# The up projection by seven block products instead of eight, in tiles of 1024 tokens

## The chip, the cores and the metric

The kernel runs on one core of a Trainium2 chip. The metric is the device time of one execution in microseconds (us). Engines are named as the profile names them: PE is TensorE (PEld its weight loads), DVE is VectorE, ACT is ScalarE, POOL is GpSimd, SP is SyncE, which issues the DMAs.

## What is computed

```python
def _attn_ref(x, f_logit, lower_bound):          # x: (2, 6080, 256)
    sig = 1.0 / (1.0 + np.exp(-f_logit))
    f = lower_bound + (1.0 - lower_bound) * sig
    i = 1.0 - f
    for t in range(S):
        h = f[:, t] * h + i[:, t] * x[:, t]
        y[:, t] = h

def _moe_ref(x, w_in, w_out):                    # 12160 tokens, 256 -> 2048 -> 256
    h = x @ w_in
    relu6 = np.clip(h + 3.0, 0.0, 6.0)
    return (h * relu6 / 6.0) @ w_out
```

A gated scan over the tokens of each of two sequences gives the states; they go through an up projection, a gate and a down projection. The inputs are float32.

## The kernel before

Channels lie on the partitions, tokens along the free dimension. The 256 channels are two groups of 128 (k = 0, 1), the 2048 hidden units sixteen blocks f of 128, the output channels two groups d. A tile is 512 tokens of one of the two sequences b (448 in each sequence's first tile), 24 tiles in all, the sequences taking turns.

To keep float32 accuracy with matmuls that round their operands, each operand is split in two: ACT casts it to the rounded type (`_hi`), and a subtraction gives the rest (`_lo`). A product is then three matmuls: hi x hi, hi x lo, lo x hi. So a tile has for each f 2 x 3 matmuls up (`up`, L436, matmuls on L449) and 2 x 3 down (`down`, L455, L469).

For each tile DVE and ACT make the states: sigmoid on ACT (L316), forget gate, drive and scan on DVE (L341, L346, L353), the cast on ACT (L321), the rest on POOL (L245, one pass over both groups). For each f, ACT clips h from below (L267, `clipped`, reads PSUM), DVE clips it from above and multiplies it with h (L363, `g`, one input in SBUF, one in PSUM), ACT casts g (L272), and DVE makes the rest (L368, both inputs in SBUF). At the tile's end ACT copies y out of PSUM (L328) and SP stores it.

PSUM holds four banks of h (`h_ps`, `SLOTS`) and four of y. The order of the work on each engine is written out by hand: TensorE does down(f) of a tile and then up(f + 4), so that four h banks lie between its two uses, and a result of `up` has about three f to pass through ACT and DVE. The work for the next tile's states is put at f = 0 to 5. Each engine takes its instructions strictly in this order; a wait on a semaphore holds everything behind it. SP loads tile t + 2 once tile t's x and z are read, from buffers for both sequences.

At the start the weights come in eight pieces of two f each and are split: casts on ACT (L258, L262), rests of w_in on DVE and POOL (L336, L235), of w_out on POOL (L229); 28 small matmuls on zeros run ahead of the first real one. The loop over the tiles is a hardware loop except for the first two and the last two tiles.

## Time and profile before

| | |
|---|---|
| median of 3 runs | 1053.38 us (1053.21 to 1053.45) |
| the profiled execution | 1055.17 us, span of its trace 1053.2 us |
| instructions | 12791, of them 4636 matmuls (28 on zeros) |
| granted TensorE clock | 0.998 of 2.4 GHz |
| DMA | 41.74 MB, 40 GB/s |
| ACT idle until a result of `up` | 504.1 us |
| DVE idle until ACT's clip | 418.2 us |

The page gives busy time and its share of the span for each engine, then the span in 40 equal slices, then a chain of waits followed back from the last instruction, then groups of instructions by line with the mean length of one in ns, the idle time of the engine just before them, and who ended it. The timeline lists instructions by start and length, with the idle time before them and its releaser in brackets.

### The profile page before, as it was taken

What the parts mean: (1) busy time and instruction counts of PE and PEld (TensorE: products, weight loads), DVE (VectorE), ACT (ScalarE), POOL (GpSimd) and SP (SyncE); (2) the same over time, 40 slices, a digit from 0 to 9 for tenths busy, and PEclk for the clock granted to TensorE, in tenths of its full rate; (3) what the DMA queues carried; (4) which work ended last, traced back from release to release, by engine and by line L of the source; (5) the groups of instructions that cost most, each with busy time, mean ns of one, the idle gap of its engine ahead of it and who ended that gap; (6) DMA issues with size and microseconds to landing.
All of it is one profiled execution on the core that took longest, in us unless ns stands there. A gap on an engine that the chain in (4) does not pass through costs nothing.

```text
span 1053.2 us, 12791 instructions
## 1 busy us (share of the span) xinstructions
PE 1044.3 (99%) x4636; PEld 870.5 (83%) x4636; DVE 623.8 (59%) x950; ACT 533.7 (51%) x859; POOL 70.7 (7%) x37
## 2 busy tenths in 40 slices
PE   7999999999999999999999999999999999999998
PEld 6998888888888888888888888888888888888887
DVE  7864665656646566465665656646556465564644
ACT  5655444544545545455454554544545544454443
POOL 3300000000000000000000000000000000000000
PEclk9999999999999999999999999999999999999999
DMA  7011010110101101011010110101101011010000
GB/s 270 1 58 44 15 61 0 60 59 1 60 0 60 60 0 60 0 60 60 0 60 0 60 60 0 60 0 60 60 0 60 17 43 60 0 60 21 1 21 20
DMA packets 22093, 41.74 MB, mean 40 GB/s; under 512 B 1600, under 2 KB 3136, under 8 KB 22080
## 3 DMA queue, kind: packets, MB, share of 16 engines
q1 hardware_dynamic: 22080, 41.56, 11.6%
q8 instruction: 9, 0.15, 0.1%
q14 instruction: 4, 0.03, 0.0%
HBM read 29.10 MB, written 12.45 MB: 39 GB/s over the span
## 4 chain that ended last, share of the span: by engine, by line
PE 98%; DVE 0%; ACT 0%; issue 0%; ACTq 0%
PE y_ps L469 49%; PE h_ps L449 49%; DVE state L353 0%; DVE state_lo L383 0%; ACT clipped L267 0%; DVE g_lo L368 0%; DVE g L363 0%; DVE drive L346 0%; ACT y_sb L328 0%; ACT g_hi L272 0%; ACT state_hi L281 0%; ACTq L266 0%
## 5 line engine op out<-in xcount | busy, mean ns | idle before, releaser
L267 ACT ACTIVATE clipped<-h_ps,half 128x512 f32<-128x512 f32 (+1 forms) x384 | 263.1, 685 | 504.1 <-PE h_ps L449 504.1
L363 DVE SCALAR_TENSOR_TENSOR g<-clipped,h_ps 128x512 f32<-128x512 f32 (+1 forms) x384 | 262.1, 683 | 418.5 <-ACT clipped L267 418.2
L449 PE MATMUL h_ps<-state_hi,w_in_hi 128*128 128x512 f32 (+1 forms) x768 | 298.3, 388 | 3.5 <-DVE state_lo L383 3.0
L469 PE MATMUL y_ps<-g_hi,w_out_hi 128*128 128x512 f32 (+1 forms) x768 | 297.4, 387 | 1.0 <-DVE g_lo L368 1.0
L449 PE MATMUL h_ps<-state_lo,w_in_hi 128*128 128x512 f32 (+1 forms) x768 | 298.1, 388 | 0.0
L449 PE MATMUL h_ps<-state_hi,w_in_lo 128*128 128x512 f32 (+1 forms) x768 | 298.0, 388 | 0.0
L469 PE MATMUL y_ps<-g_hi,w_out_lo 128*128 128x512 f32 (+1 forms) x768 | 297.4, 387 | 0.0
L469 PE MATMUL y_ps<-g_lo,w_out_hi 128*128 128x512 f32 (+1 forms) x768 | 297.4, 387 | 0.0
L368 DVE TENSOR_TENSOR g_lo<-g,g_hi 128x512 fp32r<-128x512 f32 (+1 forms) x384 | 273.4, 712 | 0.2
L272 ACT CAST g_hi<-g 128x512 fp32r<-128x512 f32 (+1 forms) x384 | 233.3, 608 | 1.2 <-DVE g L363 1.1
L449 PEld LDWEIGHTS h_ps<-state_hi,w_in_hi 128*128 128x128 f32 x768 | 144.5, 188 | 33.2 <-DVE state_lo L383 3.0
L469 PEld LDWEIGHTS y_ps<-g_hi,w_out_hi 128*128 128x128 f32 x768 | 144.1, 188 | 30.0 <-issue 1.3
L449 PEld LDWEIGHTS h_ps<-state_hi,w_in_lo 128*128 128x128 f32 x768 | 144.5, 188 | 28.8
L449 PEld LDWEIGHTS h_ps<-state_lo,w_in_hi 128*128 128x128 f32 x768 | 144.4, 188 | 28.6
L469 PEld LDWEIGHTS y_ps<-g_lo,w_out_hi 128*128 128x128 f32 x768 | 144.2, 188 | 28.9
L469 PEld LDWEIGHTS y_ps<-g_hi,w_out_lo 128*128 128x128 f32 x768 | 144.2, 188 | 28.5
L245 POOL TENSOR_TENSOR state_lo<-state,state_hi 128x1024 fp32r<-128x1024 f32 (+1 forms) x23 | 55.4, 2407 | 885.7 <-ACT state_hi L321 885.7
L353 DVE TENSOR_TENSOR_SCAN state<-gate,carry,drive 128x512 f32<-128x512 f32 (+1 forms) x48 | 61.7, 1286 | 0.2
L346 DVE SCALAR_TENSOR_TENSOR drive<-sig,one_minus_lb,x_sb 128x512 f32<-128x512 f32 (+1 forms) x48 | 35.6, 741 | 1.3 <-DMA x_sb<-in_x 1.3
L328 ACT COPY y_sb<-y_ps 128x1024 f32<-128x1024 f32 (+2 forms) x24 | 23.8, 993 | 3.4 <-PE y_ps L469 3.4
L321 ACT CAST state_hi<-state 128x1024 fp32r<-128x1024 f32 (+1 forms) x23 | 24.1, 1048 | 0.7 <-DVE state L353 0.7
L316 ACT ACTIVATE sig<-z_sb 128x1024 f32<-128x1024 f32 (+1 forms) x23 | 24.4, 1059 | 0.0
(23 smaller groups left out, 76.8 us busy)
## 6 DMA issues: line engine op xcount, KB each, us to landing
z_sb<-in_z SPq DMA_DIRECT2D x22, 512.0 KB, 4.6
x_sb<-in_x SPq DMA_DIRECT2D x22, 512.0 KB, 5.2
out_y<-y_sb SPq DMA_DIRECT2D x21, 512.0 KB, 3.2
w_in_raw<-in_w_in SPq DMA_DIRECT2D x8, 256.0 KB, 6.2
w_out_raw<-in_w_out SPq DMA_DIRECT2D x8, 256.0 KB, 7.4
out_y<-y_sb SPq DMA_DIRECT2D x2, 448.0 KB, 3.3
out_y<-y_sb SPq DMA_DIRECT2D x2, 256.0 KB, 2.1
z_sb<-in_z SPq DMA_DIRECT2D x2, 224.0 KB, 3.5
```

The lines of the kernel that those rows point to most:

```text
L245: nc.gpsimd.tensor_tensor(state_lo[:, nb, :, 0:n], state[:, :, 0:n], state_hi[:, nb, :, 0:n].bitcast(F32), ALU.subtract).then_inc(state_lo ...
L267: nc.scalar.activation(clipped[:, s, 0:n], h_ps[:, s, 0:n], ACT.Relu, bias=half[:], scale=1.0 / 6.0).then_inc(clipped_ready, 1)
L272: nc.scalar.copy(g_hi[:, s, 0:n], g[:, s, 0:n]).then_inc(g_hi_ready, 1)
L316: nc.scalar.activation(sig[:, :, 0:n], z_sb[:, nb, :, 0:n], ACT.Sigmoid, scale=-1.0).then_inc(sig_ready, 1)
L321: nc.scalar.copy(state_hi[:, nb, :, 0:n], state[:, :, 0:n]).then_inc(state_hi_ready, 1)
L328: nc.scalar.copy(y_sb[:, b, k:K, 0:n], y_ps[:, b, k:K, 0:n]).then_inc(y_copied, 1)
L346: nc.vector.scalar_tensor_tensor(drive[:, k, 0:n], sig[:, k, 0:n], one_minus_lb[:, k:k + 1], x_sb[:, b, k, 0:n], ALU.mult, ALU.mult).then_ ...
L353: nc.vector.tensor_tensor_scan(state[:, k, 0:n], gate[:, k, 0:n], drive[:, k, 0:n], carry[:, b, k:k + 1], ALU.mult, ALU.add).then_inc(stat ...
L363: nc.vector.scalar_tensor_tensor(g[:, s, 0:n], clipped[:, s, 0:n], 1.0, h_ps[:, s, 0:n], ALU.min, ALU.mult).then_inc(g_ready, 1)
L368: nc.vector.tensor_tensor(g_lo[:, s, 0:n], g[:, s, 0:n], g_hi[:, s, 0:n].bitcast(F32), ALU.subtract).then_inc(g_lo_ready, 1)
L449: last = nc.tensor.matmul(h_ps[:, s, 0:n], w[:, f, k, :], v[:, b, k, 0:n], start=(k == 0 and m == 0), stop=(k == K - 1 and m == len(terms) ...
L469: last = nc.tensor.matmul(y_ps[:, b, d, 0:n], w[:, f, at], v[:, s, 0:n], start=(f == 0 and m == 0), stop=(f == F - 1 and m == len(terms) - 1))
```

## The change

The up projection of a pair of hidden blocks (f, f + 1), the two channel groups and two halves of the tokens is a 2 x 2 block product; it is done with Strassen's method in Winograd's form, seven products instead of eight. A tile is now 1024 tokens (960 in the first two), 12 in all, and a block q is one pair of f of one tile, 96 in all.

- **Operands.** Seven weight operands per pair: three are blocks of w_in as they are, and four are sums and differences of its blocks, made by POOL at the start (`sum_w7`, four passes of 128 columns per pair), cast by ACT and completed by POOL in passes of 896 columns. Seven token operands per tile: three are states, four are sums T1 to T4 of states, and all seven are cast on ACT (`round_op`) and completed on POOL (`rest_of_op`): 11 POOL passes of 512 per tile. In tile 0 DVE takes part of these.
- **Halves.** The halves of the tokens are interleaved in runs of four tokens, so the passes over states, and the copies into y, step over every other run of 16 bytes.
- **Products.** P1 and its successors P6 and P5 are accumulated in one PSUM bank; ACT copies the bank's partial sum to SBUF after each (`copy_p1`, `copy_p16`, `copy_p165`) before TensorE adds the next. P7 and P4 share a second bank, P2 has a third. DVE adds PSUM to the copies (`add_c11`, `add_c22`, `add_c21`) and so gets three of the four blocks of h in SBUF; the fourth, C12, stays in PSUM.
- **Gate.** The gate works as before on the four blocks; for three of them both of DVE's inputs are now in SBUF. Clip and gate are in place in `g`.
- **Down.** 24 matmuls per block as before; those of block q - 1 are placed between the products of block q.
- **States.** One buffer for z, x, gate, drive and state; scans of 1024 tokens as two of 512. The load of tile t + 1 waits on SP for all operands of tile t, and stands behind the store of y of tile t - 1.
- **Loops.** Every engine's program is unrolled over all tiles.
- **Start and end.** 36 instead of 28 matmuls on zeros; the last y is copied in four parts and stored in two of 512 KB.

The core of the diff:

```diff
-            for k in range(K):
-                for f in range(LEAD):
-                    up(0, 0, f, groups=(k,))
...
-                for f in range(F):
-                    down(t, b, i, f)
-                    v = f + LEAD
-                    if exists(t, v):
-                        up(t + v // F, (b + v // F) % B, v % F)
...
+            for q in range(LAST + 1):
+                n = half_span(q // BLOCKS)
+                bank = x_ps[:, q % 2]
+                product(q, A11_B11, bank, True, n).then_inc(p1_ready, 1)
+                if q > 0:
+                    down_both(q - 1, C11)
+                pe.wait_ge(p1_copied, q + 1)
+                product(q, S2_T2, bank, False, n).then_inc(p16_ready, 1)
+                product(q, A12_B21, z_ps, True, n).then_inc(p2_ready, 1)
+                if q > 0:
+                    down(q - 1, C22, 0)
+                pe.wait_ge(p16_copied, q + 1)
+                product(q, S1_T1, bank, False, n).then_inc(p165_ready, 1)
+                if q > 0:
+                    pe.wait_ge(h_ready[C21], q)
+                product(q, S3_T3, v_ps, True, n).then_inc(p7_ready, 1)
+                if q > 0:
+                    down(q - 1, C22, 1).then_inc(down_done[C22], 1)
+                    down(q - 1, C21, 0)
+                pe.wait_ge(h_ready[C22], q + 1)
+                product(q, A22_T4, v_ps, False, n).then_inc(p74_ready, 1)
+                if q > 0:
+                    down(q - 1, C21, 1).then_inc(down_done[C21], 1)
+                pe.wait_ge(p165_copied, q + 1)
+                product(q, S4_B22, bank, False, n).then_inc(c12_ready, 1)
+                if q > 0:
+                    down_both(q - 1, C12)
...
+            def product(q, o, out, start, n):
+                t, j = divmod(q, BLOCKS)
+                b = t % B
+                if j == 0:
+                    pe.wait_ge(op_ready[o], t + 1)
+                if t == 0:
+                    pe.wait_ge(w7_ready, j + 1)
+                nc.tensor.matmul(out[:, 0:n], w7_hi[:, j, o], op_hi[:, b, o, 0:n], start=start, stop=False,
+                                 skip_group_check=True)
+                nc.tensor.matmul(out[:, 0:n], w7_hi[:, j, o], op_lo[:, b, o, 0:n], start=False, stop=False,
+                                 skip_group_check=True)
+                return nc.tensor.matmul(out[:, 0:n], w7_lo[:, j, o], op_hi[:, b, o, 0:n], start=False, stop=True,
+                                        skip_group_check=True)
...
+                    copy_p1(q, n)
+                    if j == 1 and t > 0:
+                        copy_y(t - 1, SECOND, 0)
+                    if j == 1:
+                        round_g(q - 1, C21, n)
+                        round_g(q - 1, C12, n)
+                    if t + 1 < TILES:
+                        if j in (2, 3):
+                            make_sig(t + 1, j - 2)
+                        if j == 4:
+                            round_op(t + 1, A11_B11)
+                        if j == (5 if t > 0 else 6):
+                            round_op(t + 1, S1_T1)
+                        if j == 6:
+                            round_op(t + 1, A12_B21)
+                            round_op(t + 1, S4_B22)
+                        if j == 7:
+                            round_op(t + 1, S2_T2)
+                            round_op(t + 1, S3_T3)
+                    copy_p16(q, n)
+                    if j == 1 and t > 0:
+                        copy_y(t - 1, SECOND, 1)
+                    clip_lower(q, C11, n)
+                    copy_p165(q, n)
+                    round_g(q, C11, n)
+                    if t == 0 and j + 2 < BLOCKS:
+                        round_w_out(j + 2)
+                    clip_lower(q, C22, n)
+                    round_g(q, C22, n)
+                    if j == 0 and t > 0:
+                        copy_y(t - 1, FIRST, 0)
+                        copy_y(t - 1, FIRST, 1)
+                    if t == 0 and j + 2 < BLOCKS:
+                        round_w7(j + 2)
+                    if j == 7 and t + 1 < TILES:
+                        round_op(t + 1, A22_T4)
+                    clip_lower(q, C21, n)
+                    clip_lower(q, C12, n)
+                    if j != 0:
+                        round_g(q, C21, n)
...
+            def copy_p16(q, n):
+                act.wait_ge(p16_ready, q + 1)
+                if q > 0:
+                    act.wait_ge(g_ready[C21], q)
+                nc.scalar.copy(h_sb[:, C21, 0:n], x_ps[:, q % 2, 0:n]).then_inc(p16_copied, 1)
...
+            def add_c11(q, n):
+                dve.wait_ge(p2_ready, q + 1)
+                dve.wait_ge(p1_copied, q + 1)
+                nc.vector.tensor_tensor(h_sb[:, C11, 0:n], z_ps[:, 0:n], h_sb[:, C11, 0:n],
+                                        ALU.add).then_inc(h_ready[C11], 1)
...
+            def gate_h(q, u, n):
+                dve.wait_ge(clipped_ready[u], q + 1)
+                h = x_ps[:, q % 2, 0:n] if u == C12 else h_sb[:, u, 0:n]
+                nc.vector.scalar_tensor_tensor(g[:, u, 0:n], g[:, u, 0:n], 1.0, h,
+                                               ALU.min, ALU.mult).then_inc(g_ready[u], 1)
+
+            def rest_of_g(q, u, n):
+                dve.wait_ge(g_hi_ready[u], q + 1)
+                nc.vector.tensor_tensor(g_lo[:, u, 0:n], g[:, u, 0:n], g_hi[:, u, 0:n].bitcast(F32),
+                                        ALU.subtract).then_inc(g_lo_ready[u], 1)
...
+                    q = t * BLOCKS + j
+                    if t + 1 < TILES:
+                        if j == 2:
+                            make_drive(t + 1, 0)
+                            make_gate(t + 1, 0)
+                        if j == 3:
+                            scan(t + 1, 0)
+                        if j == 4:
+                            make_drive(t + 1, 1)
+                            make_gate(t + 1, 1)
+                        if j == 5:
+                            scan(t + 1, 1)
+                        if j == 6:
+                            for k in range(K):
+                                keep_carry(t + 1, k)
+                    add_c11(q, n)
+                    gate_h(q, C11, n)
+                    add_c22(q, n)
+                    rest_of_g(q, C11, n)
+                    gate_h(q, C22, n)
+                    add_c21(q, n)
+                    rest_of_g(q, C22, n)
+                    gate_h(q, C21, n)
+                    gate_h(q, C12, n)
+                    rest_of_g(q, C21, n)
+                    rest_of_g(q, C12, n)
...
+            def sum_w7(j):
+                raw = w7_raw[:, j]
+                pool.wait_ge(w_in_loaded[j], 16)
+                nc.gpsimd.tensor_tensor(raw[:, S1_T1], raw[:, 2], raw[:, 3], ALU.add).then_inc(w7_sums_ready, 1)
+                pool.wait_ge(w7_sums_ready, 4 * j + 1)
+                nc.gpsimd.tensor_tensor(raw[:, S2_T2], raw[:, S1_T1], raw[:, 0], ALU.subtract).then_inc(w7_sums_ready, 1)
+                nc.gpsimd.tensor_tensor(raw[:, S3_T3], raw[:, 0], raw[:, 2], ALU.subtract).then_inc(w7_sums_ready, 1)
+                pool.wait_ge(w7_sums_ready, 4 * j + 3)
+                nc.gpsimd.tensor_tensor(raw[:, S4_B22], raw[:, 1], raw[:, S2_T2], ALU.subtract).then_inc(w7_sums_ready, 1)
+
+            def rest_of_w7(j):
+                pool.wait_ge(w7_hi_ready, j + 1)
+                nc.gpsimd.tensor_tensor(w7_lo[:, j], w7_raw[:, j], w7_hi[:, j].bitcast(F32),
+                                        ALU.subtract).then_inc(w7_ready, 1)
...
+                if t + 1 < TILES:
+                    T, n = t + 1, half_span(t + 1)
+                    make_t1(T)
+                    rest_of_op(T, A11_B11)
+                    rest_of_op(T, S1_T1)
+                    pool.wait_ge(state_ready[1], 2 * (T + 1))
+                    pool.wait_ge(t1_ready, T + 1)
+                    nc.gpsimd.tensor_tensor(packed(t_b, n), state_half(1, SECOND, n), packed(t_a, n),
+                                            ALU.subtract).then_inc(t2_ready, 1)
+                    nc.gpsimd.tensor_tensor(packed(t_c, n), state_half(1, SECOND, n), state_half(0, SECOND, n),
+                                            ALU.subtract).then_inc(t3_ready, 1)
+                    rest_of_op(T, A12_B21)
+                    rest_of_op(T, S4_B22)
+                    pool.wait_ge(t2_ready, T + 1)
+                    pool.wait_ge(op_ready[S1_T1], T + 1)
+                    nc.gpsimd.tensor_tensor(packed(t_a, n), state_half(1, FIRST, n), packed(t_b, n),
+                                            ALU.subtract).then_inc(t4_ready, 1)
+                    rest_of_op(T, S2_T2)
+                    rest_of_op(T, S3_T3)
+                    rest_of_op(T, A22_T4)
...
+            for t in range(TILES):
+                if t + 1 < TILES:
+                    for o in range(PRODUCTS):
+                        sp.wait_ge(op_ready[o], t + 1)
+                    sp.wait_ge(carry_ready, K * (t + 1) + B * K)
+                    for k in range(K):
+                        load(t + 1, k)
+                n = 2 * half_span(t)
+                if t < TILES - 1:
+                    sp.wait_ge(y_copied[FIRST], K * (t + 1))
+                    sp.wait_ge(y_copied[SECOND], K * (t + 1))
+                    sp.dma_start(tokens_of(y, t), y_sb[:, :, 0:n]).then_inc(y_stored, 16)
```

## Rows read from the trace of the kernel before

**Rows 1.** The page's busy time per engine, and the granted clock in 40 slices.

```profile
PE 1044.3 (99%) x4636; PEld 870.5 (83%) x4636; DVE 623.8 (59%) x950; ACT 533.7 (51%) x859; POOL 70.7 (7%) x37
...
PEclk9999999999999999999999999999999999999999
```

**Rows 2.** The page's chain that ended last: shares of the span by engine.

```profile
PE 98%; DVE 0%; ACT 0%; issue 0%; ACTq 0%
```

**Rows 3.** Timeline: start, duration, engine, line; PE at 512 columns, then at 448.

```profile
502.95 0.39 PE L449 MATMUL h_ps<-state_hi,w_in_lo 128*128 128x512 f32 x1
...
505.67 0.39 PE L449 MATMUL h_ps<-state_hi,w_in_lo 128*128 128x512 f32 x1
...
20.43 0.37 PE L469 MATMUL y_ps<-g_hi,w_out_hi 128*128 128x448 f32 x1
...
22.91 0.37 PE L469 MATMUL y_ps<-g_hi,w_out_hi 128*128 128x448 f32 x1
```

**Rows 4.** Timeline: ACT and DVE behind the matmul that starts at 502.95.

```profile
503.37 0.69 ACT L267 ACTIVATE clipped<-h_ps,half 128x512 f32<-128x512 f32 x1 [1.52 <-PE h_ps L449]
...
503.96 0.61 ACT L272 CAST g_hi<-g 128x512 fp32r<-128x512 f32 x1
...
504.10 0.69 DVE L363 SCALAR_TENSOR_TENSOR g<-clipped,h_ps 128x512 f32<-128x512 f32 x1 [0.23 <-ACT clipped L267]
...
504.70 0.69 DVE L368 TENSOR_TENSOR g_lo<-g,g_hi 128x512 fp32r<-128x512 f32 x1
```

**Rows 5.** Timeline: how soon TensorE goes on when it waited for DVE.

```profile
17.10 0.63 DVE L368 TENSOR_TENSOR g_lo<-g,g_hi 128x448 fp32r<-128x448 f32 x1
...
17.88 0.44 PE L469 MATMUL y_ps<-g_hi,w_out_hi 128*128 128x448 f32 x1 [0.98 <-DVE g_lo L368]
...
18.16 0.36 PE L469 MATMUL y_ps<-g_lo,w_out_hi 128*128 128x448 f32 x1
```

**Rows 6.** Groups of instructions by shape: busy us, mean ns, idle before, releaser.

```profile
L353 DVE TENSOR_TENSOR_SCAN state<-gate,carry,drive 128x512 f32<-128x512 f32 x44 | 56.3, 1279 | 0.0
...
L346 DVE SCALAR_TENSOR_TENSOR drive<-sig,one_minus_lb,x_sb 128x512 f32<-128x512 f32 x44 | 32.8, 746 | 0.0
...
L316 ACT ACTIVATE sig<-z_sb 128x1024 f32<-128x1024 f32 x22 | 23.4, 1064 | 0.0
...
L341 DVE TENSOR_SCALAR gate<-sig,lb_minus_one 128x512 f32<-128x512 f32 x44 | 21.2, 481 | 0.0
```

**Rows 7.** Timeline of POOL: two single passes, and two back to back.

```profile
9.42 3.71 POOL L235 TENSOR_TENSOR w_in_lo<-w_in_raw,w_in_hi 128x512 fp32r<-128x512 f32 x2 [8.97 <-ACT w_in_hi L258]
...
24.79 1.29 POOL L229 TENSOR_TENSOR w_out_lo<-w_out_raw,w_out_hi 128x512 fp32r<-128x512 f32 x1 [5.31 <-ACT w_out_hi L262]
...
508.32 2.40 POOL L245 TENSOR_TENSOR state_lo<-state,state_hi 128x1024 fp32r<-128x1024 f32 x1 [41.12 <-ACT state_hi L321]
```

**Rows 8.** Timeline of DVE beside the POOL passes of rows 7.

```profile
10.06 1.99 DVE L353 TENSOR_TENSOR_SCAN state<-gate,carry,drive 128x448 f32<-128x448 f32 x1
...
24.85 1.49 DVE L341 TENSOR_SCALAR gate<-sig,lb_minus_one 128x448 f32<-128x448 f32 x1
...
509.54 0.69 DVE L363 SCALAR_TENSOR_TENSOR g<-clipped,h_ps 128x512 f32<-128x512 f32 x1 [1.35 <-ACT clipped L267]
510.14 1.13 DVE L368 TENSOR_TENSOR g_lo<-g,g_hi 128x512 fp32r<-128x512 f32 x1
```

**Rows 9.** The page's DMA issues: KB each, median us from issue to landing.

```profile
z_sb<-in_z SPq DMA_DIRECT2D x22, 512.0 KB, 4.6
x_sb<-in_x SPq DMA_DIRECT2D x22, 512.0 KB, 5.2
out_y<-y_sb SPq DMA_DIRECT2D x21, 512.0 KB, 3.2
```

**Rows 10.** Timeline: the first matmul of the up projection, and ACT's last copy.

```profile
9.06 0.47 PE L449 MATMUL h_ps<-state_hi,w_in_hi 128*128 128x448 f32 x1 [2.79 <-DVE state_lo L383]
...
1050.09 0.59 ACT L328 COPY y_sb<-y_ps 128x512 f32<-128x512 f32 x1 [3.37 <-PE y_ps L469]
```

More of the change, by code:

```diff
@@ L40 @@
 N = 512
+ROW = 2048
+SMALL_FROM = 16512
 ALU = mybir.AluOpType
@@ L44 @@
 F32R = mybir.dt.float32r
-SLOTS = 4
-LEAD = SLOTS
-WG = 2
-WARM_UP = 28
+U8 = mybir.dt.uint8
+RUN = 4
+WARM_UP = 36
 WARM_N = 256
-ROW = 2048
-PAD_FROM = 16512
+A11_B11, A12_B21, S3_T3, A22_T4, S1_T1, S2_T2, S4_B22 = range(7)
+PRODUCTS = 7
+C11, C22, C21, C12 = range(4)
+UNITS = 4
+FIRST, SECOND = 0, 1
 def build(nc, x, z, lb, w_in, w_out, y):
@@ L498 @@
+            for d in range(K):
+                down(LAST, C11, d)
+                down(LAST, C21, d).then_inc(down_done[C21], 1)
+            for d in range(K):
+                down(LAST, C22, d)
+                down(LAST, C12, d).then_inc(y_tail_ready, 1)
 def kernel(x, f_logit, lower_bound, moe_w_in, moe_w_out):
```

631 lines of the change are left out of this document (325 added, 306 removed).

## Prediction

> **What bounds the kernel now.** Busy time first: TensorE works 99% of the span, DVE 59%, ACT 51% [rows 1]; the chain of waits agrees, 98% of it is TensorE [rows 2]. So the time is the number of matmuls times their spacing. The timeline gives the spacing: 12 matmuls of 512 columns in 505.67 - 502.95 = 2.72 us, 0.2267 each; of 448 columns in 2.48 us, 0.2067 each [rows 3]. (The 0.39 us of a row is the length of one matmul in the pipeline.) Now 22 x 192 x 0.2267 + 2 x 192 x 0.2067 = 957.6 + 79.4 = 1037.0 us, and 16.2 us of the span of 1053.2 are start and end. The profiled execution took 1055.17, the median is 1053.38, nearly the span: I sum against the span and take the result for the median.
>
> **What is removed.** Per pair of f and 1024 tokens 7 x 3 + 24 = 45 matmuls instead of 48. There are 96 such blocks: 80 at 512 columns, 45 x 0.2267 = 10.20 us each; 16 at 480, whose spacing I interpolate to 0.2167, 9.75 us each. Together 816.1 + 156.0 = 972.1, **64.9 us less**. What remains is whether the other engines let TensorE run so.
>
> **The plain block.** Before, ACT and DVE stood beside the path: four h banks lay between them and TensorE. Now TensorE waits inside each block for three copies of ACT and one addition of DVE. Prices of a handoff: the matmul that starts at 502.95 releases ACT at 503.37 (0.42 from start to start); ACT ends at 504.06, DVE starts at 504.10 (0.04); back to back, DVE starts an instruction every 0.60 and ACT every 0.59 although one lasts 0.69 [rows 4]. TensorE goes on 0.22 after DVE's end: g_lo ends at 17.73, and the second matmul at 18.16, less one spacing, puts the first at 17.95 [rows 5]. A plain copy out of PSUM takes 0.59 [rows 10], a cast 0.61 [rows 4]; the three new additions read PSUM and SBUF as L363 does, so 0.69; the clips of C11, C22, C21 read SBUF, near 0.63. ACT gets 11 passes a block instead of 8, DVE 11 instead of 8.
>
> With time 0 at the start of S2_T2's product: its and P2's last matmul starts at 1.13, add_c11 1.55, clip C11 2.28, gate C11 2.95, add_c22 3.55 to 4.24, TensorE may start A22_T4 at 4.46. By its own order it gets there after 21 matmuls, at 4.76: **0.30 us of slack**. The rest of the chain (gate C22 5.0, add_c21 5.6, rest C22 6.4, gate C21 7.0, gate C12 7.7, round C12 8.45, next copy_p1 9.03 to 9.62) allows the next block at 9.84 where TensorE needs 10.20: slack 0.36. So plain blocks run at TensorE's pace, but anything over 0.3 us late on DVE stops TensorE, and such a stop is never won back.
>
> **What is late in a tile.** Besides the 88 passes DVE has per tile two drives of 1024 (746 ns + 512/0.96 = 1.28), two gates (481 + 267 = 0.75) and four scans (1.28) [rows 6], 9.2 us. They stand ahead of add_c11, where DVE is free from 9.70 to 11.75, 2.05 us.
> - j=2: sig (1.06 [rows 6]) ends 0.48 after time 0, then drive and gate to 2.5: add_c11 0.95 late, stop 0.65.
> - j=3: two scans, the second behind the first: stop 0.25.
> - The load of the next tile is queued on SP behind the store of the last one, which waits for copy_y in j=1. From about 14.5 us into the tile 1 MB of y, then z, then x must land. 512 KB of y land in 3.2, z and x together in 5.7 [rows 9], so x comes about 9 us later, at 23.5, where drive wants it at 22.9: +0.6, between 0 and 3.
>
> **The shared price: POOL.** POOL gets 11 passes of 512 per tile, 1.29 each (1024 take 2.40) [rows 7], 14 us instead of 4.8 for the same tokens; my estimate of a pass is 0.18 + 2.2 per 1024. They are off the path by themselves. But look at DVE beside POOL: g_lo, two SBUF inputs, takes 1.13 instead of 0.69 and ends at 511.27, POOL ended at 510.72; the gate takes 1.49 instead of 0.45 and ends at 26.34, POOL at 26.08; the scan at 10.06 takes 1.99; but L363 at 509.54, one input in PSUM, keeps its 0.69 [rows 7, 8]. So a DVE pass that reads only SBUF waits until POOL's pass ends, and the two passes of POOL at 9.42, 3.71 instead of 2.58, wait for DVE in turn: they alternate [rows 7]. The new block makes this worse: gates of C11, C22, C21 now read SBUF alone, 7 of 11 passes instead of 4 of 8 can be held up, and the slack is 0.3, where the old loop could hide all of it.
>
> The Trainium skill (SBUF — State Buffer, "SBUF: two separate sides") has the same as a rule: the pair of ports that both engines share is locked for a whole instruction, and the loser blocks. By that rule, the trace agrees, the loss is to be counted in whole POOL passes and not as a few per cent of bandwidth.
>
> Stops from it, block by block. j=4: POOL's rest of A11 gets in between drive and gate, DVE 0.94 late, 0.6. j=5: it gets in between the two scans (add_c11 1.5 late, 1.2, of which 0.2 DVE's own), then t_c holds the rest of C11: 0.2 more. j=6: t4, at 2.6 to 3.9, holds gate C11 for 0.95: 0.5. j=7: the round of A22 delays the clip of C21, and POOL's rest of A22 then holds its gate to 8.24: next copy_p1 0.95 late, 0.7. With j=2, j=3 and the load: 0.65 + 0.25 + 0.6 + 0.6 + 1.4 + 0.5 + 0.7 = 4.7, and 0.1 at the tile's start for the moved y copies: **4.8 us per tile, 48 us in tiles 1 to 10**; tile 11 prepares nothing.
>
> **Start, tile 0, end.** Now the first up matmul starts at 9.06 [rows 10] and 12.8 of the 16.2 us are lost ahead and around it. New: k=0 needs 960 tokens instead of 448 (drive, gate, two scans, 4.3 instead of 2.3), POOL makes four sums and the rest of 896 weights (4 x 0.46 + 2.1), then t1 and A11's rest (1.2 each): first product near 16. The second half of the channels, then eight DVE passes, alternating with POOL: block 1 starts near 31, with 21 matmuls (4.6) done. Lost 27 instead of 12.8: **+14** (6 to 20). In tile 0 POOL has 5.3 us of weight passes per block and ACT 0.93 + 0.51 in the chain; released by that rounding, POOL's 2.1 us pass lands on gate C21: about 2.2 a block, six times; then POOL, late, does tile 1's 11 passes in j=6 and 7, where ACT waits for t1 in its order: 6. **+19** (6 to 30). End: the last units' g_lo (0.4) and a store twice as large: +1.5.
>
> Sum: 972.1 + 16.2 + 14 + 19 + 48 + 1.5 = 1070.8; since not every stop adds to the one before it (a late block gives POOL more room) I take a tenth off the 67 of stops: **1064**.
>
> What costs nothing: strided passes in runs of four floats. No row has such a pass; there are some 15 per tile (four of POOL's sums, the rounds and rests that read the states, the y copies). Bounds: 0, and, if each ran at half speed, 0.5 us more each, 7.5 per tile, 80 us in all. I take 0, the plain passes' rows being the nearest.
> The Trainium skill (SBUF — State Buffer, "Door 1: The DMA port swizzle") says that a 16-byte line read whole runs at full rate; four floats are such a line; no row here shows it.
> The unrolled program: the page's loops show no gap, tiles outside the loop neither; 0.
>
> **Rivals.**
> - Faster: the POOL passes fall into DVE's free 2 us or are won back. For it: DVE has 20% free. Against it: the order puts them behind ACT's rounds, which start just as drive and scan do. Time: 972.1 + 16.2 + 14 + 1.5, per tile 1.5, tile 0 5: 1024. With half of the stops 1042. Chance 0.36 that it ends below 1051.
> - Slower than forecast, the same side: handoffs with two or three semaphores cost more than the 0.04 measured; from 0.04 more at each of the ten in the chain the plain block is no longer TensorE's; at 0.08 it is 10.6, 96 x 0.4 = 38 on top, less what it hides: 1090. Chance 0.12. The load that lands 3 us late: +24, 1088. Chance 0.05.
> - Strided passes at half speed: half of those 80 us in stops, 1104. Chance 0.05.
> My own case, 1045 to 1085, holds what remains, 0.42; nearly all of it lies over 1055.5. A change under 0.2% (2 us) is what a measurement of this kernel can't tell from none; that narrow band gets 0.04. Faster 0.37, same 0.04, slower 0.59. The range, 1020 to 1094, leaves the strided case and the best of the faster one out.
>
> **What would show it.** Plain blocks (j=1) 10.2 us apart; TensorE idle before the products A22_T4 and S2_T2, released by DVE additions and by copy_p1, about 5 us in each tile and none in the last; g_lo and gates of over 1.1 us beside POOL; block 1 at about 31. Wrong, if TensorE is busy without gaps in j=4 to 7, or if gaps stand in j=1 too.

## The result, and the profile after

The changed kernel takes 1103.87 us (median of 4 runs, 1102.16 to 1107.14), the kernel before on the same chip 1053.41: a ratio of 1.0478, interval 1.0463 to 1.0493. It is slower, the side that was forecast, but by 50.5 us and not by 10.6, and it lies beyond the range's upper end of 1094. The profiled execution took 1102.24 with a span of 1100.5, 47.3 more than the span before.

The page after: busy time, granted clock, and the chain's shares by engine.

```profile
PE 1018.1 (93%) x4356; PEld 823.4 (75%) x4356; DVE 861.7 (78%) x1190; ACT 739.8 (67%) x1229; POOL 232.0 (21%) x176
...
PEclk7899999999999999999999999999999999999999
...
DVE 35%; PE 30%; ACT 18%; issue 13%; DMA 2%; POOL 1%; SPq 0%; ACTq 0%; DVEq 0%; POOLq 0%
```

Beside [rows 1, 2]: 4356 matmuls instead of 4636, but TensorE is down to 93% and the chain, once 98% TensorE, now runs for more than half (53%) over DVE and ACT. The waits say who holds TensorE (columns: who waited at which line for what: us in total, times, longest):

```profile
PE v_ps L566 <- DVE h_sb L467: 39.4, 47, 2.2
...
PE x_ps L566 <- ACT h_sb L311: 25.0, 19, 8.3
...
PE x_ps L566 <- POOL op_lo L227: 10.9, 1, 10.9
```

The first line is the product A22_T4 waiting for DVE's add_c22: 47 stops. The second is S2_T2, a block's second product, waiting for copy_p1. The third is the very first product, waiting for POOL's rest of its operand.

**The account of the span.** I take the start of add_c11 (L461) in each block as the clock of the loop. Work 972.1 us (96 blocks of 45 matmuls); 31.2 lost until block 1 begins at 35.7; 24.9 in the rest of tile 0 (add_c11 goes from 42.53 in its block 1 to 132.36 in the first block of tile 1); 67.4 in tiles 1 to 10, of which tiles 3 to 10 lose about 7.1 each; none in tile 11; 4.9 at the end. The sum is 1100.5. Three windows show the stages (columns: stretch, length, then busy us (instructions) of PE, PEld, DVE, ACT, POOL, then PEclk, DMA share, GB/s):

```profile
0.00:40.00 40.00, 17.60 (x70) 14.61 (x71) 26.99 (x31) 16.84 (x26) 23.92 (x25) 0.74 0.57 203
40.00:120.00 80.00, 65.00 (x267) 52.25 (x266) 65.43 (x80) 49.02 (x84) 50.03 (x39) 0.94 0.00 1
300.00:900.00 600.00, 571.84 (x2435) 459.17 (x2434) 480.31 (x666) 413.48 (x684) 99.98 (x72) 0.99 0.10 37
```

The number of matmuls in the third is the better reading: without stops 600 us hold 600/0.2267 = 2646, here 2435, so 211 x 0.2267 = 48 us are lost in 6.8 tiles. (Busy time understates a stop, since the last matmul before it still counts for its whole length.)

**The plain block** keeps TensorE's pace. DVE in tile 11, which prepares nothing:

```profile
1063.15 0.69 DVE L461 TENSOR_TENSOR h_sb<-z_ps,h_sb 128x512 f32<-128x512 f32 x1 [1.87 <-PE z_ps L570]
1064.63 0.69 DVE L479 SCALAR_TENSOR_TENSOR g<-g,h_sb 128x512 f32<-128x512 f32 x1 [0.79 <-ACT g L332]
1065.24 0.68 DVE L467 TENSOR_TENSOR h_sb<-v_ps,h_sb 128x512 f32<-128x512 f32 x1
...
1073.35 0.69 DVE L461 TENSOR_TENSOR h_sb<-z_ps,h_sb 128x512 f32<-128x512 f32 x1 [1.87 <-PE z_ps L570]
```

The blocks are 10.20 apart, to the hundredth. add_c22 ends at 1065.92, 4.32 after time 0 (1063.15 - 1.55 = 1061.60); with 0.22 TensorE may start A22_T4 at 4.54, where its order brings it at 4.76: slack 0.22, not 0.30.

**A steady tile** (t=5), the matmuls behind TensorE's stops. First a short stop, in j=2, then the long one, in j=5, and last the long one of tile 7:

```profile
503.02 0.39 PE L589 MATMUL y_ps<-g_hi,w_out_lo 128*128 128x512 f32 x1
503.84 0.50 PE L566 MATMUL v_ps<-op_hi,w_hi 128*128 128x512 f32 x1 [0.43 <-DVE h_sb L467]
504.18 0.39 PE L568 MATMUL v_ps<-op_lo,w_hi 128*128 128x512 f32 x1
...
535.82 0.39 PE L589 MATMUL y_ps<-g_hi,w_out_lo 128*128 128x512 f32 x1
538.36 0.80 PE L566 MATMUL v_ps<-op_hi,w_hi 128*128 128x512 f32 x1 [2.15 <-DVE h_sb L467]
538.95 0.63 PE L568 MATMUL v_ps<-op_lo,w_hi 128*128 128x512 f32 x1
539.38 0.63 PE L570 MATMUL v_ps<-op_hi,w_lo 128*128 128x512 f32 x1
...
541.51 0.53 PE L568 MATMUL x_ps<-op_lo,w_hi 128*128 128x512 f32 x1
541.88 0.40 PE L570 MATMUL x_ps<-op_hi,w_lo 128*128 128x512 f32 x1
...
716.07 0.50 PE L566 MATMUL v_ps<-op_hi,w_hi 128*128 128x512 f32 x1 [2.15 <-DVE h_sb L467]
716.41 0.40 PE L568 MATMUL v_ps<-op_lo,w_hi 128*128 128x512 f32 x1
716.64 0.39 PE L570 MATMUL v_ps<-op_hi,w_lo 128*128 128x512 f32 x1
```

Starts apart, less 0.2267, give the loss. The short stop costs 0.59, and 0.11 for the matmul after it. The long one costs 2.31, and then **the matmuls are 0.427 apart and not 0.227 until 541.5**: the lower of the clock's two levels, 1.2 instead of 2.4 GHz, for another 1.7 us, 1.6 without the 0.11 that the short stop has too. **That does not follow every long stop.** Nine tiles, 2 to 10, have one of 2.12 to 2.17 us in j=5. In six (tiles 4, 5, 6, 8, 9, 10) eight slow matmuls come behind it, in tiles 8 and 9 after three or four at full speed. In three (tiles 2, 3, 7) none come, as the last lines show: the add_c11 of j=5 and j=6 are then 11.0 us apart and not 12.6. What decides between them no run shows. Read so, the stops of this tile are 0.70 (j=2), 0.50 (j=3), 0.90 (j=4), 4.0 (j=5), 0.35 (j=6), 0.61 (j=7), 0.1 at the tile's start: 7.2.

What makes the long one, POOL and DVE in j=5:

```profile
531.56 1.93 POOL L227 TENSOR_TENSOR op_lo<-t_a,op_hi 128x512 fp32r<-128x512 f32 x1 [9.14 <-ACT op_hi L307]
534.65 1.28 POOL L263 TENSOR_TENSOR t_b<-x_sb,t_a 128x512 f32<-128x512 f32 x1 [1.16 <-DVE x_sb L443]
535.89 1.27 POOL L265 TENSOR_TENSOR t_c<-x_sb 128x512 f32<-128x512 f32 x1
```

```profile
531.12 1.28 DVE L440 TENSOR_TENSOR_SCAN x_sb<-z_sb,carry,x_sb 128x512 f32<-128x512 f32 x1
532.43 2.14 DVE L443 TENSOR_TENSOR_SCAN x_sb<-z_sb,x_sb 128x512 f32<-128x512 f32 x1
534.49 0.66 DVE L461 TENSOR_TENSOR h_sb<-z_ps,h_sb 128x512 f32<-128x512 f32 x1
535.94 1.76 DVE L479 SCALAR_TENSOR_TENSOR g<-g,h_sb 128x512 f32<-128x512 f32 x1 [0.79 <-ACT g L332]
537.62 0.68 DVE L467 TENSOR_TENSOR h_sb<-v_ps,h_sb 128x512 f32<-128x512 f32 x1
```

POOL's rest gets between the two scans (it waits itself, 1.93 instead of 1.29, and then holds the second scan, 2.14 instead of 1.28). t_c, back to back with t_b, starts 0.05 before the gate of C11 and holds it: 1.76 instead of 0.69. add_c11 at 534.49, with one input in PSUM, keeps its 0.66 beside t_b. Over the whole run the same line of the kernel shows it (by shape; busy us, mean ns):

```profile
L479 DVE SCALAR_TENSOR_TENSOR g<-g,h_sb 128x512 f32<-128x512 f32 x240 | 187.3, 781 | 78.9 <-ACT g L332 77.1
...
L479 DVE SCALAR_TENSOR_TENSOR g<-g,x_ps 128x512 f32<-128x512 f32 x80 | 54.5, 681 | 4.8 <-ACT g L332 4.8
```

One operation, two sources: 781 ns from SBUF, 681 from PSUM.

### The profile page after: what moved, and what is told of

Read it like the earlier page. It is cut to its first block, busy times and chain, and to the rows that moved or that the text cites. A ratio compares the mean times of both kernels' runs of the same rounds, so it can differ in the third digit from the quotient of the medians.

```text
span 1100.5 us, 12941 instructions
## 1 busy us (share of the span) xinstructions
PE 1018.1 (93%) x4356; PEld 823.4 (75%) x4356; DVE 861.7 (78%) x1190; ACT 739.8 (67%) x1229; POOL 232.0 (21%) x176
## 4 chain that ended last, share of the span: by engine, by line
DVE 35%; PE 30%; ACT 18%; issue 13%; DMA 2%; POOL 1%; SPq 0%; ACTq 0%; DVEq 0%; POOLq 0%
DVE g L479 14%; DVE g_lo L484 9%; ACT g_hi L339 8%; ACT g L332 6%; PE y_ps L587 5%; PE y_ps L588 5%; PE y_ps L589 5%; DVE h_sb L461 5%; PE x_ps L566 3%; PE x_ps L568 3%; PE x_ps L570 3%; DVE x_sb L426 3%; DVE x_sb L440 3%; DMA x_sb<-in_x 2%; PE v_ps L566 2%
## 5 line engine op out<-in xcount | busy, mean ns | idle before, releaser
L479 DVE SCALAR_TENSOR_TENSOR g<-g,h_sb 128x512 f32<-128x512 f32 (+1 forms) x288 | 230.6, 801 | 101.0 <-ACT g L332 99.0
L332 ACT ACTIVATE g<-h_sb,half 128x512 f32<-128x512 f32 (+1 forms) x288 | 207.4, 720 | 128.0 <-DVE h_sb L461 126.4
L566 PE MATMUL x_ps<-op_hi,w_hi 128*128 128x512 f32 (+1 forms) x384 | 154.2, 402 | 36.8 <-ACT h_sb L311 25.0
L568 PE MATMUL x_ps<-op_lo,w_hi 128*128 128x512 f32 (+1 forms) x384 | 151.3, 394 | 0.0
L570 PE MATMUL x_ps<-op_hi,w_lo 128*128 128x512 f32 (+1 forms) x384 | 150.6, 392 | 0.0
L566 PEld LDWEIGHTS x_ps<-op_hi,w_hi 128*128 128x128 f32 x384 | 73.6, 192 | 60.7 <-ACT h_sb L311 33.3
L566 PE MATMUL v_ps<-op_hi,w_hi 128*128 128x512 f32 (+1 forms) x192 | 81.8, 426 | 40.0 <-DVE h_sb L467 39.4
L461 DVE TENSOR_TENSOR h_sb<-z_ps,h_sb 128x512 f32<-128x512 f32 (+1 forms) x96 | 64.9, 676 | 66.3 <-PE z_ps L570 66.3
L570 PEld LDWEIGHTS x_ps<-op_hi,w_lo 128*128 128x128 f32 x384 | 73.7, 192 | 15.1
L568 PEld LDWEIGHTS x_ps<-op_lo,w_hi 128*128 128x128 f32 x384 | 73.8, 192 | 14.1
```

The source lines that it names most:

```text
L332: nc.scalar.activation(g[:, u, 0:n], h, ACT.Relu, bias=half[:], scale=1.0 / 6.0).then_inc(clipped_ready[u], 1)
L461: nc.vector.tensor_tensor(h_sb[:, C11, 0:n], z_ps[:, 0:n], h_sb[:, C11, 0:n], ALU.add).then_inc(h_ready[C11], 1)
L479: nc.vector.scalar_tensor_tensor(g[:, u, 0:n], g[:, u, 0:n], 1.0, h, ALU.min, ALU.mult).then_inc(g_ready[u], 1)
L566: nc.tensor.matmul(out[:, 0:n], w7_hi[:, j, o], op_hi[:, b, o, 0:n], start=start, stop=False, skip_group_check=True)
L568: nc.tensor.matmul(out[:, 0:n], w7_hi[:, j, o], op_lo[:, b, o, 0:n], start=False, stop=False, skip_group_check=True)
L570: return nc.tensor.matmul(out[:, 0:n], w7_lo[:, j, o], op_hi[:, b, o, 0:n], start=False, stop=True, skip_group_check=True)
```

## The experiments

**My theory** after this reading: the tiles' stops are DVE passes that POOL's passes hold up, laid on preparation passes that alone already fill DVE's free time, and where both come together the stop is long and the clock can fall behind it. **Rivals:** the handoffs are too dear whatever the preparation does; POOL's passes slow TensorE or the rest of the chain by themselves, by their busy time; the start and tile 0 carry the loss.

**1. POOL's passes nearly taken away.** In tiles 1 to 11 POOL's 11 passes work on 32 tokens instead of 512; the remainders and sums of the other tokens are left out.

```diff
-                n = half_span(t)
+                n = half_span(t) if t == 0 else SHORT
...
-                    T, n = t + 1, half_span(t + 1)
+                    T, n = t + 1, SHORT
```

> POOL's 11 passes of tiles 1 to 11 work on 32 tokens instead of 512 (the rests and sums of the other tokens are left out), all waits and all work of DVE, ACT and TensorE stay. The lock theory (a POOL pass holds DVE's SBUF-only passes, and slack is 0.3 us): stops in tiles 1 to 10 fall from 6.7 us a tile to about 2.5, those of blocks j=2, 3 and 0, and no stop is long enough for the clock to fall: 1104 - 42 - 5 (tile 0's end) = near 1057, between 1050 and 1065. The rival (DVE's own added work and ACT's roundings in the chain are what is late): nearly nothing is gained, 1090 to 1104.

**2. DVE's preparation nearly taken away.** Drive, gate and scan of tiles 1 to 11 work on 64 of 1024 tokens; the states of the others are left out. **3.** Both together.

```diff
-                n = 2 * half_span(t)
+                n = 2 * half_span(t) if t == 0 else 2 * S_SHORT
...
-                b, n = t % B, half_span(t)
+                b, n = t % B, half_span(t) if t == 0 else S_SHORT
```

> DVE's drive, gate and scan of tiles 1 to 11 work on 64 of 1024 tokens (the states of the rest are left out); POOL's passes stay at 512. The lock theory: j=2 and 3 lose their stops, and POOL's passes in j=4 and 5 fall into DVE's free time; those that hit gates (t_b, t_c, t4, the rest of A22) stay, 1.5 to 2.5 us a tile: 1050 to 1065. The rival (DVE is short of time by itself): the same as with short POOL passes on top, under 1045.

> Both of the above. Both theories: nearly no stops in tiles 1 to 11, blocks 10.2 us apart; what is left is start and tile 0: 1104 - 67 - 5 to 8, 1029 to 1040. If it stays over 1050, ACT's roundings and the copies of y are a cause of their own.

Measured: 1052.23 without POOL's passes (ratio 0.9982, 0.9972 to 0.9991), 1047.31 without DVE's (0.9946, 0.9926 to 0.9965), 1027.93 without both (0.9754, 0.9738 to 0.9771). The first lies in its range; the second lies between the theory's range and the rival's, the third 1.1 us below its range. Windows of the three, 300 to 900:

```profile
300.00:900.00 600.00, 593.06 (x2587) 482.67 (x2586) 476.89 (x703) 437.89 (x726) 28.23 (x77) 1.00 0.12 43
```

```profile
300.00:900.00 600.00, 594.73 (x2597) 485.51 (x2596) 447.29 (x708) 440.70 (x729) 97.67 (x77) 1.00 0.12 43
```

```profile
300.00:900.00 600.00, 600.00 (x2646) 495.83 (x2645) 440.46 (x722) 448.79 (x741) 19.29 (x79) 1.00 0.11 41
```

The third is without a gap, 2646 matmuls, so the rival of the handoffs falls: the block's 22 chained passes cost nothing of themselves. Left per tile (the start of add_c11 in tiles 3 to 11, less the work) are 2.0 us with DVE's preparation alone and 1.7 with POOL's alone; 3.7 as a sum, but 7.1 together. **Nearly half of the loss belongs to neither, only to their meeting**, and the clock's 1.6 in six of the tiles is in that part: in all three runs the granted clock of the stretch is 1.00, after the change 0.99. The third also shows what the change was worth with tiles that prepare for nothing: 25 us, near the 1024 of the "faster" rival.

**4. Shorter POOL passes.** Each of the 11 passes of tiles 1 to 11 as two of half the tokens, with one semaphore count for both.

```diff
-                nc.gpsimd.tensor_tensor(packed(t_a, n), state_half(0, SECOND, n), state_half(0, FIRST, n),
-                                        ALU.subtract).then_inc(t1_ready, 1)
+                difference(t, t_a, state_half(0, SECOND, n), state_half(0, FIRST, n), n).then_inc(t1_ready, 1)
...
+                parts = (slice(0, 2 * cut),) if t == 0 else (slice(0, cut), slice(cut, 2 * cut))
+                for r in parts:
+                    last = nc.gpsimd.tensor_tensor(packed(out, n)[:, r], a[:, r], b[:, r], ALU.subtract)
```

> Each of POOL's 11 passes of tiles 1 to 11 as two passes of 256 tokens: POOL's time rises from about 14 to 16 us a tile, the longest hold falls from 1.28 to 0.73 us. The lock theory: DVE gets in between the halves, stops of j=4, 5 and 6 shrink by 0.3 to 0.5 each and the long stop of j=5 goes under what lets the clock fall: 1080 to 1095. The rival (what counts is POOL's total time on the shared ports): the same or slower, 1104 to 1112.

Measured: 1067.99 (ratio 1.0132, 1.0115 to 1.0149), 36 us less than the changed kernel, more than I had expected of it. The window, POOL's busy time fourth from the end, and DVE and POOL in j=5:

```profile
300.00:900.00 600.00, 587.66 (x2544) 473.60 (x2544) 483.16 (x694) 431.45 (x714) 137.19 (x154) 1.00 0.10 38
```

```profile
520.67 1.58 DVE L449 TENSOR_TENSOR_SCAN x_sb<-z_sb,x_sb 128x512 f32<-128x512 f32 x1
522.17 0.66 DVE L467 TENSOR_TENSOR h_sb<-z_ps,h_sb 128x512 f32<-128x512 f32 x1
523.62 1.10 DVE L485 SCALAR_TENSOR_TENSOR g<-g,h_sb 128x512 f32<-128x512 f32 x1 [0.80 <-ACT g L338]
```

POOL works more, 137 us against 100, and everything gets faster: busy time is not what counts, and how long one pass holds DVE fits. The scan takes 1.58 instead of 2.14, the gate 1.10 instead of 1.76, the longest stop of TensorE in tiles 1 to 10 is 1.1 instead of 2.2, and the clock stays at 1.00. About 10 of the 36 us are the six falls of the clock that no longer come (6 x 1.6), the rest shorter stops. This speaks for the theory and against the rival by which POOL's busy time counts.

**5. The start.** ACT makes copy_p1 of block 0 right after the round of A12_B21, not behind the last roundings.

```diff
+            copy_p1(0, half_span(0))
...
-                    copy_p1(q, n)
+                    if q > 0:
+                        copy_p1(q, n)
```

> ACT's first copy of P1 is put ahead of the last roundings of tile 0's operands and of the second weights' rounding, behind which it stood (TensorE idle 8.35 us until it). The theory that this order is part of the longer start: the second product starts about 4 us earlier, and 3 to 5 us are gained: 1099 to 1101. The rival (the start is set by the operands and POOL's weight passes): the wait only moves, 1103 to 1104.

Measured: 1100.92 (ratio 1.0456, 1.0439 to 1.0474), span 1100.4. The long wait of 8.3 us is gone, and add_c11 of block 0 starts at 27.06 instead of 31.44; but by the first block of tile 1 only 0.9 of these 4.4 us are left (131.48 against 132.36), and nothing of them at the end. The median lies in the range of the theory, but the ratio intervals overlap and the profiled spans are nearly the same (1100.4 and 1100.5): no gain that I can tell. The wait only moved, into tile 0; that POOL's weight passes set the pace there is argued, not shown by this run.

**6. POOL passes where nothing is tight.** The kernel before, with four more passes of 512 on spare buffers in each tile.

```diff
+                    for v in range(4):
+                        if v > 0 or not (isinstance(t, int) and t == 0):
+                            pool.wait_ge(spare_ready, t * 4 + v)
+                        nc.gpsimd.tensor_tensor(spare[:], zeros[:], zeros[:], ALU.subtract).then_inc(spare_ready, 1)
```

> The kernel before, with four more POOL passes of 512 per tile of 512 tokens on spare buffers, behind state_lo: POOL then works 15 us per 1024 tokens, as much as in the changed kernel. The theory that the thin slack makes the lock costly: g_lo takes over 1.1 us in more places, TensorE waits for none of it, and the time stays within 0.3% of 1053.4. The rival (POOL's passes cost TensorE time wherever they are): from 10 us more, 1063 and over.

Measured: 1058.05 (ratio 1.0037, 1.0023 to 1.0051), a little over the 0.3% that I had expected, and far from the rival's 1063. Window 440 to 700, and the one stop that costs it:

```profile
440.00:700.00 260.00, 260.00 (x1149) 215.29 (x1148) 155.99 (x234) 130.88 (x209) 43.83 (x30) 1.00 0.11 36
```

```profile
45.60 0.74 PE L479 MATMUL y_ps<-g_hi,w_out_hi 128*128 128x448 f32 x1 [2.64 <-POOL w_out_lo L233]
```

In the steady state TensorE is busy throughout with POOL at 17%, as much as after the change (100 of 600): POOL by itself is not the cause. POOL beside TensorE costs nothing; beside a DVE with 0.2 us of slack it does. The 3.4 us of span come from one stop in tile 0, where the weights' remainder queued behind the added passes: it costs 2.8 itself, and the matmuls behind it stand 0.37 apart at 448 columns instead of 0.21, until 48.8.

**7. Shorter still.** Four passes of a quarter.

```diff
+            def parts(t, n):
+                m = 1 if t == 0 else PIECES
+                return [slice(i * n // RUN // m, (i + 1) * n // RUN // m) for i in range(m)]
```

> Each of POOL's 11 passes of tiles 1 to 11 as four of 128 tokens (about 0.46 us each, 20 us of POOL a tile in place of 14). The lock theory, stops set by the length of one hold: on from 1068 with halves (3.6 us of stops a tile) towards the 2.2 a tile that 32-token passes left: 1055 to 1062. The rival (the fixed cost of a pass and the number of changes of hand count): slower again than halves, 1070 or more.

Measured: 1067.65 (ratio 1.0128, 1.0112 to 1.0145), the same as halves, and in neither range: the theory's 1055 to 1062 was wrong, and nothing got slower either. POOL is busy 177.8 of 600 us there. Each hold is shorter and there are more of them; I did not separate the two, so that they cancel is only argued.

**8. DVE's preparation spread.** Passes of full length, but one or two of them ahead of each block's add_c11 in j=2 to 6 (the drive of the second channels in two halves, the scans one by one), the sigmoids and roundings of ACT placed accordingly, and the load put ahead of the store on SP.

```diff
                         if j == 3:
-                            scan(t + 1, 0)
+                            scan_first(t + 1, 0)
+                            make_drive(t + 1, 1, 0)
                         if j == 4:
-                            make_drive(t + 1, 1)
-                            make_gate(t + 1, 1)
+                            scan_second(t + 1, 0)
+                            make_drive(t + 1, 1, 1)
```

> POOL's passes whole. DVE's state passes of the next tile in five blocks (j=2 drive and gate of k=0; j=3 first scan and half of k=1's drive; j=4 second scan, the other half; j=5 gate and scan; j=6 scan), none over the 2.05 us that DVE has free; ACT's sigmoids and two of its roundings moved to its free places, SP loads ahead of the store. The theory that DVE's own late passes are 2.2 us a tile and that they meet POOL's: 2.2 and part of the 3.4 that only both together cost go: 1050 to 1075. The rival (only the length of POOL's holds counts): 1090 or more.

**9. Spread, and POOL in halves,** with the weights' remainders in tile 0 cut as well (896 into 256, 256, 256, 128; 512 into two).

```diff
-                nc.gpsimd.tensor_tensor(w7_lo[:, j], w7_raw[:, j], w7_hi[:, j].bitcast(F32),
-                                        ALU.subtract).then_inc(w7_ready, 1)
+                for o in (slice(0, 2), slice(2, 4), slice(4, 6), slice(6, 7)):
+                    last = nc.gpsimd.tensor_tensor(w7_lo[:, j, o], w7_raw[:, j, o], w7_hi[:, j, o].bitcast(F32),
+                                                   ALU.subtract)
+                last.then_inc(w7_ready, 1)
```

> c2 with POOL's token passes in halves, and the weight passes of tile 0 cut too (896 columns into 256, 256, 256, 128; 512 into two of 256). Expected by the lock theory: stops in tiles 1 to 10 under 2 a tile, tile 0 shorter by 5 to 10 us: 1025 to 1045, below the kernel before. If tile 0 stays as it is, its stops come from ACT's weight roundings in the chain, and the time is 1040 to 1050.

Measured: 1067.23 (1.0129, 1.0112 to 1.0145) for the spread alone, 1056.54 (1.0023, 1.0013 to 1.0034) with the halves. The first is in its range, the second misses it by over 11 us (1025 to 1045): 2.45 us of stops a tile are left, not under 2, and add_c11 of tile 1's first block comes 3.8 us earlier (128.60 instead of 132.36), not 5 to 10. Each of the two cures alone takes some 36 us off, both, with the cut weight passes, 47: they cure partly the same thing. What is left per tile in the ninth is mostly one stop, in j=7, the matmul that waits for copy_p1 while POOL works without a break:

```profile
533.96 0.50 PE L594 MATMUL x_ps<-op_hi,w_hi 128*128 128x512 f32 x1 [1.27 <-ACT h_sb L325]
```

**10, 11. The clock, by itself.** In the kernel before, TensorE waits once per tile for a POOL pass on spare buffers: 512 elements, or 832.

```diff
+                pool.wait_ge(stop_asked, t)
+                nc.gpsimd.tensor_tensor(spare[:, 0:512], zeros[:, 0:512], zeros[:, 0:512], ALU.subtract
+                                        ).then_inc(stop_over, 1)
...
+                    if f == 10 and not (isinstance(t, int) and t == 0):
+                        pe.wait_ge(stop_over, t)
```

> The kernel before, in which TensorE waits once in each tile but the first (23 times) for a POOL pass of 512 that its own last matmul released: a stop of 0.42 + 1.3 + 0.2 - 0.2, about 1.8 us, made on purpose. The time of the stops alone: 23 x 1.8 = 41, 1095. The theory that a stop costs more than its length when the granted clock falls behind it: then the matmuls behind the stop show a spacing of 0.43 instead of 0.227; whether 1.8 us is long enough for it isn't known from the traces (1.3 was not, 2.3 was). The rival (a stop costs its length): spacing 0.227 at once.

> The same with a POOL pass of 832, a stop of about 2.5 us. Length alone: 23 x 2.5 = 58, 1112. With the clock's fall behind each stop, eight matmuls at 0.43 as in the changed kernel (1.6 us more a stop): 58 + 37 = 95, 1149. The rival: 1112, spacing 0.227 at once.

Measured: 1098.39 (ratio 1.0427, 1.041 to 1.0445) and 1141.59 (1.0839, 1.082 to 1.0857). There are 23 stops, so 45.0/23 = 1.96 us and 88.2/23 = 3.83 us each. Behind a stop of the first, then of the second:

```profile
491.97 0.50 PE L463 MATMUL h_ps<-state_hi,w_in_hi 128*128 128x512 f32 x1 [1.64 <-POOL spare L263]
492.31 0.39 PE L463 MATMUL h_ps<-state_lo,w_in_hi 128*128 128x512 f32 x1
492.54 0.40 PE L463 MATMUL h_ps<-state_hi,w_in_lo 128*128 128x512 f32 x1
```

```profile
506.99 0.64 PE L463 MATMUL h_ps<-state_hi,w_in_hi 128*128 128x512 f32 x1 [2.17 <-POOL spare L263]
507.43 0.63 PE L463 MATMUL h_ps<-state_lo,w_in_hi 128*128 128x512 f32 x1
...
510.42 0.49 PE L483 MATMUL y_ps<-g_hi,w_out_lo 128*128 128x512 f32 x1
```

The idle time grew by 0.53 us, the mean cost by 1.87. After 1.64 us of idle time TensorE goes on at 0.227 in all 23 tiles, and the granted clock of the run is 0.998; after 2.17, eight matmuls stand 0.43 apart in 19 of the 23 tiles and none in four, and the granted clock is 0.970. The sum comes out: 23 stops at the length of 2.5 (1.96 + 0.53) and 19 times 1.6 make 88. That is the picture of the changed kernel's j=5, without the holds on DVE or the block products in it: the slow matmuls come with the longer stop and with nothing else that was changed.

**12. The version from all of it.** On the ninth, POOL is held back until DVE's last remainder of a block is done, so that its passes fall where DVE has only PSUM passes or nothing; in tile 0 the weights' remainders wait likewise, their sums are made two pairs ahead, and ACT's rounding of them goes behind copy_p16. What each of these edits brings was not separated.

```diff
+            def after_rests(t, j):
+                if t > 0:
+                    pool.wait_ge(g_lo_ready[C21], t * BLOCKS + j + 1)
...
+                    pool.wait_ge(state_ready[1], 2 * T + 1)
                     rest_of_op(T, A11_B11)
+                    after_rests(t, 5)
                     rest_of_op(T, S1_T1)
```

> The last variant (spread state passes, halves on POOL) with POOL held back: its passes for the next tile wait for DVE's rest of C21 in j=5, 6 and 7, behind which DVE is nearly idle for 3 us, and so do the weight passes of tile 0; ACT's weight rounding of tile 0 stands in its free place behind copy_p16. The lock theory: stops of 2.45 us in a tile go to about 1.2 (12 us), tile 0 from 18 us of stops to 8 to 12: 1034 to 1040, 1.5% faster than the kernel before. The rival (tile 0's stops come from ACT's and DVE's work there, not from where POOL's passes fall): 1045 to 1050.

Measured: 1042.47 (1042.08 to 1042.58), ratio 0.9893, 0.9876 to 0.9909: **1.1% faster than the kernel before**, between its expectation and the rival's.

```profile
40.00:120.00 80.00, 74.26 (x325) 60.69 (x323) 68.21 (x93) 58.56 (x101) 53.65 (x68) 0.98 0.00 1
300.00:900.00 600.00, 593.76 (x2601) 485.81 (x2600) 495.19 (x717) 438.63 (x729) 135.37 (x154) 1.00 0.10 39
```

In tile 0, 325 matmuls where the changed kernel has 267; in the steady stretch 2601 instead of 2435. Per steady tile 1.5 us of stops are left (83.13 between the add_c11 of the same block in two tiles, less 81.60), 16.5 in ten tiles instead of 67: the start and tile 0 were not the main cause of the loss, but they are the largest rest now, some 47 of the 68.7 us that the span of 1040.8 has over the work. The start wasn't worked on further.

## Why the prediction was right or wrong

- **Work, 972.1: right.** Blocks 10.20 apart in tile 11, and no gap in 600 us in the third run.
- **The plain block: right, its slack a little too large.** 0.22 instead of 0.30. The term that was off was the clip from SBUF, "near 0.63"; it takes 0.72 as a mean (busy us, mean ns):

```profile
L332 ACT ACTIVATE g<-h_sb,half 128x512 f32<-128x512 f32 (+1 forms) x288 | 207.4, 720 | 128.0 <-DVE h_sb L461 126.4
```

- **POOL's hold on DVE: the right mechanism.** Passes reading only SBUF are held, those with an input in PSUM are not. The Trainium skill (SBUF — State Buffer, "SBUF: two separate sides") says that the port pair is an exclusive lock for a whole instruction, and that a DVE operation with two SBUF inputs contends only with a GpSimd one that reads SBUF; by that rule, the trace agrees, with the gate's 1.76 against add_c11's 0.66. Run 4 measures it: halving the unit of the lock recovered 36 us, about 10 of them through the clock, although POOL's busy time rose.
- **Stops of a tile, 4.8: measured 7.2 in tile 5, 6.7 as the mean of tiles 1 to 10; this is the step that failed, and in it j=5.** Forecast and measured (tile 5): j=2 0.65 and 0.70, j=3 0.25 and 0.50, j=4 0.6 and 0.90, **j=5 1.4 and 4.0**, j=6 0.5 and 0.35, j=7 0.7 and 0.61, the load 0.6 and nearly nothing, the tile's start 0.1 and 0.1. That add_c11 of j=5 would be 1.5 late was nearly right: it is 1.66 late (534.49, where 532.83 was due). What I gave to t_c, "holds the rest of C11: 0.2 more", was wrong: it holds the gate, which stands ahead of add_c22, and add_c22 starts 3.13 after add_c11 instead of 2.09, so 1.04. With the smaller slack that makes 2.5 instead of 1.4. The rest of the 4.0 is the clock.
- **The clock was not in the sum at all.** A stop was priced at its length. Behind six of the nine stops of some 2.15 us the granted clock is at its lower level for eight matmuls, 1.6 us more each, and about 10 us in all. TensorE never stopped in the loop of the kernel before, but its start had the warning. Behind the 2.79 us of idle time of [rows 10] come six matmuls at full speed and 0.59 us more of idle time, and from 11.15 on the matmuls of 448 columns stand 0.37 apart and not 0.2067:

```profile
11.52 0.57 PE L449 MATMUL h_ps<-state_lo,w_in_hi 128*128 128x448 f32 x1
11.89 0.57 PE L449 MATMUL h_ps<-state_hi,w_in_lo 128*128 128x448 f32 x1
```

- **"I take a tenth off the 67 of stops": wrong in sign.** Run 3 against 1 and 2 shows that late passes do not make room for each other: 2.0 and 1.7 apart give 7.1 together.
- **Start and tile 0: 27 and 19 forecast, 31.2 and 24.9 measured.** The order and the queues were right. Missed at the start: copy_p1 of block 0 stands behind the last roundings in ACT's order, and TensorE waits 8.35 for it:

```profile
28.63 0.77 PE L566 MATMUL x_ps<-op_hi,w_hi 128*128 128x480 f32 x1 [8.35 <-ACT h_sb L311]
```

Behind it, until 33.2, the matmuls of 480 columns stand 0.40 apart and not 0.2167, 1.8 us more. Run 5 shows that this wait is not worth its length. In tile 0 the hold that the prediction described can be seen: POOL's rest of 896 weights meets the gate of C21, which takes 2.09 instead of 0.66, and TensorE then waits 2.24 us for the next copy_p1:

```profile
48.59 2.13 POOL L216 TENSOR_TENSOR w_lo<-w_raw,w_hi 128x896 fp32r<-128x896 f32 x1 [4.69 <-ACT w_hi L287]
49.13 2.09 DVE L479 SCALAR_TENSOR_TENSOR g<-g,h_sb 128x480 f32<-128x480 f32 x1 [0.78 <-ACT g L332]
```

How the rest of tile 0's loss divides was not separated. The slow matmuls are no part of it that shows: they come behind three of its stops here and behind none of the first four in run 4, and those blocks are equally far apart in both (13.27, 13.71, 13.24 and 13.70 here, 13.26, 13.69, 13.23 and 13.71 there). The end, 3.4 + 1.5 = 4.9, was right.
- **The rivals.** "Handoffs cost more" is refuted by run 3. The load that lands late is hardly there: from 210 to 1010 us DVE waits 2.7 us for x in all. Strided passes cost nothing extra on POOL: t_b and t_c, which take the sums from the states, last 1.28 and 1.27, as a plain pass [rows 7]; nor on ACT, whose casts from the states take 623 ns on average and those from the packed sums 621 to 622. (They had been costed at 1104, close to what came out, by a mechanism that isn't there.) One number of the faster rival doesn't come out of its terms: 1003.8 and half of the 67 of stops make 1037, not 1042.

In numbers: the start 4.4 (31.2 less 12.8 + 14), tile 0 5.9, tiles 1 to 10 19.4 and the 6.8 of the wrong tenth make 36.5; on the forecast of 1064 that is the span, 1100.5. Of the 19.4 about half is the clock, and most of the rest is the hold on the gate in j=5, 1 us a tile. Of the last 3.4 us to the median, 1.7 lie outside the span of the profiled execution; I had taken the one for the other. The other 1.6 are the spread of the executions: this one took 1102.24, the four 1102.16 to 1107.14.

## What to carry to other kernels

Where an edit uses up an engine's slack, price the collisions of its passes with the other user of the port one by one and by where they stand in the chain; slack of 0.2 us turns each into a stop, and two lateness sources that meet cost more than their sum. Keep passes on POOL short and time them to where DVE reads PSUM: the same work in two halves won back 36 of 50 us, and with DVE's preparation spread and POOL paced a loss of 4.8% became a gain of 1.1%. A stop of TensorE can have a second price behind it: of 23 stops of 1.64 us none was followed by slow matmuls, of 23 of 2.17 us 19 were, at 1.6 us each. Look at the spacing of the matmuls after a stop, in several tiles.
